# Value product with the features on partitions, probabilities scaled on GpSimd, in a float32 attention and mixture-of-experts kernel on one Trainium2 core

## What is computed

```python
scores = scale * np.matmul(q, k.transpose(0, 1, 3, 2))
scores = np.where(masks[None, :, :, :], scores, -1000000000.0)
scores = scores - np.max(scores, axis=-1, keepdims=True)
attn = np.exp(scores)
attn = attn / (np.sum(attn, axis=-1, keepdims=True) + 1e-09)
out = np.matmul(attn, v)
...
x = attn_out.transpose(0, 2, 1, 3).reshape(B * S, H * D)
x = _moe_ref(x=x, **moe_kwargs)       # x @ w_in, h * tanh(softplus(h)), @ w_out
return _moe2_ref(x=x, **moe2_kwargs)  # one of eight experts for each row
```

## Time and profile before

| | |
|---|---|
| three runs | 965.39, 967.73, 969.03 us, median 967.73 us |
| profiled execution, first to last instruction | 966.3 us |
| busy: PE, DVE, ACT, POOL | 860.1, 766.8, 390.3, 354.2 us |
| matmuls | 5778 |

### The profile page before, as it was taken

One profiled execution on the slowest core, in us unless ns is written; L12 is line 12 of the kernel. 1 busy time (PEld: TensorE's weight loads), 2 busy tenths in 40 slices (PEclk: granted clock), 3 DMA queues, 4 the chain that ended last, 5 costly groups with the idle time before them and its releaser, 6 DMA issues.

```text
span 966.3 us, 17706 instructions
## 1 busy us (share of the span) xinstructions
PE 860.1 (89%) x5778; PEld 788.7 (82%) x5779; DVE 766.8 (79%) x1658; ACT 390.3 (40%) x1043; POOL 354.2 (37%) x281
## 2 busy tenths in 40 slices
PE   5777899999998999998899889996599999999995
PEld 4676798888988988888898889995488888888884
DVE  5899988989888888887888988775657776778752
ACT  5565454545435445454544544445131122311300
POOL 4757432333243334333334333325414324423400
PEclk9789999999999999999999999997699999999998
DMA  9332411121121112112111211203473364645210
GB/s 326 132 128 85 140 32 46 59 64 45 41 68 42 54 50 67 42 42 67 42 47 61 62 42 64 90 1 120 164 267 126 125 214 133 188 160 191 71 44 22
DMA packets 34121, 91.00 MB, mean 94 GB/s; under 512 B 4224, under 2 KB 4672, under 8 KB 34048
## 3 DMA queue, kind: packets, MB, share of 16 engines
q1 hardware_dynamic: 18608, 48.31, 15.4%
q10 hardware_dynamic: 12224, 31.46, 9.7%
q0 software_dynamic: 3216, 10.26, 3.0%
HBM read 77.65 MB, written 12.37 MB: 93 GB/s over the span
## 4 chain that ended last, share of the span: by engine, by line
PE 39%; DVE 38%; ACT 12%; issue 9%; DMA 2%; DVEq 0%; SPq 0%; POOL 0%; ACTq 0%; POOLq 0%
PE ps_h L498 13%; PE acc L517 12%; DVE u_sb L806 6%; DVE u_sb L804 5%; DVE neg_max L754 5%; ACT probs L611 5%; DVE h_sb L812 4%; PE ps_h L389 4%; DVE row_max L747 3%; DVE probs L743 3%; PE acc L404 3%; DVE g_hi L817 2%; ACT u_sb L624 2%; ACT u_sb L626 2%; PE misc L416 2%
## 5 line engine op out<-in xcount | busy, mean ns | idle before, releaser
L1084 POOL TENSOR_TENSOR g_lo<-h_sb,g_hi 128x288 fp32r<-128x288 f32 x128 | 103.0, 805 | 296.8 <-DVE g_hi L817 296.8
L404 PE MATMUL acc<-g_hi,w_hi 128*128 128x288 f32 x512 | 161.4, 315 | 0.9 <-POOL g_lo L1084 0.9
L389 PE MATMUL ps_h<-xT_hi,w_hi 128*128 128x288 f32 x512 | 158.9, 310 | 0.0
L389 PE MATMUL ps_h<-xT_hi,w_lo 128*128 128x288 f32 x512 | 155.5, 304 | 0.0
L389 PE MATMUL ps_h<-xT_lo,w_hi 128*128 128x288 f32 x512 | 155.3, 303 | 0.0
L404 PE MATMUL acc<-g_lo,w_hi 128*128 128x288 f32 x512 | 152.7, 298 | 0.0
L404 PE MATMUL acc<-g_hi,w_lo 128*128 128x288 f32 x512 | 152.2, 297 | 0.0
L624 ACT ACTIVATE u_sb<-u_sb 128x288 f32<-128x288 f32 x128 | 56.8, 444 | 180.7 <-DVE u_sb L806 178.8
L1079 POOL TENSOR_TENSOR stage_lo<-stage,qk_hi 128x704 fp32r<-128x704 f32 x52 | 88.4, 1701 | 103.8 <-ACT qk_hi L603 103.7
L611 ACT ACTIVATE probs<-probs,neg_max 72x104 f32<-72x104 f32 (+1 forms) x224 | 84.6, 379 | 98.6 <-DVE neg_max L754 98.6
L806 DVE SCALAR_TENSOR_TENSOR u_sb<-u_sb 128x288 f32<-128x288 f32 x128 | 99.6, 778 | 4.4
(11 more groups left out here) (139 smaller groups left out, 2011.5 us busy)
## 6 DMA issues: line engine op xcount, KB each, us to landing
stage<-in_pack SPq DMA_DIRECT2D x57, 480.0 KB, 3.4
stage<-in_w ACTq DMA_DIRECT2D x32, 512.0 KB, 7.8
stage_w<-in_w ACTq DMA_DIRECT2D x28, 512.0 KB
x_row<-dispatched_x SPq DMA_DIRECT2D x22, 258.0 KB, 2.6
w_loaded<-in_w_in SPq DMA_DIRECT2D x8, 512.0 KB, 5.9
w_loaded<-in_w_out SPq DMA_DIRECT2D x8, 512.0 KB, 7.1
dispatched_x<-x2T SPq DMA_DIRECT2D x8, 258.0 KB, 4.7
stage_w<-in_w SPq DMA_DIRECT2D x4, 512.0 KB
```

The costliest lines, as they stand in the source:

```text
L389: mm = pe.matmul(ps_h[f % 2][:, 0:CHUNK], w[:, o + k * PIECE:o + k * PIECE + P], x[:, par, k, :], start=(k == 0 and w is w_hi and x is xT_hi),
L404: mm = pe.matmul(acc[d][:, 0:CHUNK], w[:, o + d * P:o + (d + 1) * P], g[:, f % RING, :], start=(f == 0 and w is w_hi and g is g_hi), stop= ...
L1084: nc.gpsimd.tensor_tensor(g_lo[:, f % RING, :], h_sb[:, f % RING, :], g_hi[:, f % RING, :].bitcast(F32), ALU.subtract).then_inc(g_lo_done, 1)
```

## The change

The value product is turned round: the values (64 features of a head) are the stationary operand and `probsT` moves, so the result has features on partitions and needs no transpose. Two heads share a pair of partition halves, with the layout that the transposed `o_sb` had. Since queries are then columns, 1/sum can't be applied to the product as one number for each partition; it is applied to `probs` ahead of the transpose, by POOL (`normalise`). The transposes L377 and `o_sb` are gone. 1/sum is now made in the even step (`invert_sums`), behind that step's rounding L817 and ahead of the clamp L804, and waits for the exponentials. The PE transposes of the probabilities wait for POOL's product (`weights_ready`) where they waited for the exponentials (`probs_ready`). `misc` has one use less for each group.

```diff
             def transpose_probs(a, par, g, use):
                 nq, nk = spec(g)
-                pe.wait_ge(probs_ready, a * NG + g + 1)
+                pe.wait_ge(weights_ready, a * NG + g + 1)
...
             def values(a, g, use, bank):
+
                 nq, nk = spec(g)
                 pe.wait_ge(misc_read, use)
                 for h in range(HG):
-                    mm = pe.matmul(bank[0:nq, h * DH:(h + 1) * DH], probsT[0:nk, h * QP:h * QP + nq],
+                    half, j = h % 2 * DH, h // 2
+                    mm = pe.matmul(bank[half:half + DH, j * P:j * P + nq],
                                    group_place(qkv, w_loaded, a, g)[0:nk, V_OFF + h * DH:V_OFF + (h + 1) * DH],
-                                   start=True, stop=True, skip_group_check=True)
-                mm.then_inc(misc_full, 1)
-
-            def transpose_out(g, use, bank):
-                nq, _ = spec(g)
-                pe.wait_ge(misc_read, use)
-                for j in range(2):
-                    mm = pe.transpose(bank[:, j * P:j * P + nq], o_sb[0:nq, j * P:(j + 1) * P], ident[0:nq, 0:nq])
+                                   probsT[0:nk, h * QP:h * QP + nq], start=True, stop=True, skip_group_check=True)
                 mm.then_inc(misc_full, 1)
...
-            def normalise(a, par, g, use, bank):
+            def invert_sums(a, par, g):
                 nq, _ = spec(g)
                 G = a * NG + g
                 r = (par + g) % 2
+                dve.wait_ge(probs_ready, G + 1)
                 nc.vector.tensor_scalar(sums_eps[0:nq, r, :], sums[0:nq, r, :], 1e-9, None, ALU.add).then_inc(eps_done, 1)
                 dve.wait_ge(eps_done, G + 1)
                 nc.vector.reciprocal(rsum[0:nq, r, :], sums_eps[0:nq, r, :]).then_inc(rsum_done, 1)
-                dve.wait_ge(rsum_done, G + 1)
-                dve.wait_ge(misc_full, use + 1)
-                nc.vector.tensor_tensor(o_sb[0:nq, :].rearrange("q (h d) -> q h d", h=HG),
...
                     if mlp and (st >= 1 or later):
                         make_g(n - 1, (st - 1) % NF)
+                    if attn and st % 2 == 0 and g < NG:
+                        invert_sums(c + 1, apar, g)
                     if mlp:
                         make_n(n, st)
                     if routing and st - 1 in ROUTE_STEPS[0:3]:
                         choose(c - 1, ROUTE_STEPS.index(st - 1))
-                    if attn and st % 2 == 1 and g < NG:
-                        normalise(c + 1, apar, g, u0 + uses[("V", g)], misc)
...
+            invert_sums(0, 0, 0)
             for g in range(NG):
+                if g + 1 < NG:
+                    invert_sums(0, 0, g + 1)
                 copy_probsT(g, PROLOGUE[("T", g)])
...
+            def normalise(a, par, g):
+
+                nq, nk = spec(g)
+                r = (par + g) % 2
+                pool.wait_ge(rsum_done, a * NG + g + 1)
+                nc.gpsimd.tensor_tensor(probs[0:nq, r, :, 0:nk], probs[0:nq, r, :, 0:nk],
+                                        rsum[0:nq, r, :].unsqueeze(2).to_broadcast([nq, HG, nk]), ALU.mult
+                                        ).then_inc(weights_ready, 1)
...
                     if st >= 1 or later:
                         subtract_g(c * NF + st - 1, (st - 1) % NF)
+                    if attn and st % 2 == 0 and st // 2 < NG:
+                        normalise(c + 1, 1 - par, st // 2)
 
             W_FIRST = NG - 2
             pool.wait_ge(qk_lo_done, 2)
             for g in range(NG):
+                normalise(0, 0, g)
                 if g + 2 < NG:
                     subtract_qk(0, 0, g + 2)
```

More of the change, by code:

```diff
@@ L66, in misc_uses @@
     for st in range(NF):
-        if attn and st % 2 == 0 and 1 <= st // 2 <= NG:
-            order.append(("X", st // 2 - 1))
         if route and st in ROUTE_STEPS:
@@ L73, in misc_uses @@
     return {u: i for i, u in enumerate(order)}
-PROLOGUE = {u: i for i, u in enumerate([("T", 0), ("V", 0)] + [(u, h) for g in range(1, NG) for u, h in
-                                                                (("T", g), ("X", g - 1), ("V", g))] + [("X", NG - 1)])}
+PROLOGUE = {(u, g): 2 * g + i for g in range(NG) for i, u in enumerate("TV")}
 def build(nc, pack, masks, eye, tri, small, gates, w_in, w_out, w1, w2, out):
@@ L123, in build @@
         probsT = sb("probsT", [P, HG * QP], F32, phase1)
-        o_sb = sb("o_sb", [QP, HG * DH], F32, phase1)
         pad_rows = x2T[:, 1:3, :].rearrange("p r n -> p (r n)")[:, 0:ROW]
@@ L184, in build @@
         rsum_done = sem("rsum_done")
+        weights_ready = sem("weights_ready")
         misc_full = sem("misc_full")
@@ L233, in uses_before @@
             if isinstance(c, int) and c == 0:
-                return len(ROUTE)
-            return 2 * len(ROUTE) - len(SUB) + len(SUB) * c
+                return len(PROLOGUE)
+            return len(PROLOGUE) + len(ROUTE) - len(SUB) + len(SUB) * c
         row_banks = [ps_h[0][0:TT, :], ps_h[1][0:TT, :], ps_s[0:TT, :, :].rearrange("p h k -> p (h k)")]
-        TAIL_BASE = 2 * len(ROUTE) + (NCHUNK - 2) * len(SUB) + len(TAIL)
+        TAIL_BASE = len(PROLOGUE) + len(ROUTE) + (NCHUNK - 2) * len(SUB) + len(TAIL)
         def group_place(ring, weights, a, g):
@@ L437, in round_ @@
                         gemm1(c, par, st)
-                    if attn and st % 2 == 0 and 1 <= g <= NG:
-                        transpose_out(g - 1, u0 + uses[("X", g - 1)], misc)
                     if attn and st % 2 == 1 and g < NG:
@@ L454, in _ @@
             for g in range(NG):
-                transpose_probs(0, 0, g, PROLOGUE[("T", g - 1)] + 1 if g else None)
+                transpose_probs(0, 0, g, PROLOGUE[("T", g)] - 1 if g else None)
                 if g + 2 < NG:
                     scores(0, 0, g + 2)
-                if g:
-                    transpose_out(g - 1, PROLOGUE[("V", g - 1)] + 1, ps_h[(g - 1) % 2])
                 values(0, g, PROLOGUE[("T", g)] + 1, acc[g % 2])
-            transpose_out(NG - 1, PROLOGUE[("V", NG - 1)] + 1, ps_h[(NG - 1) % 2])
             pe.wait_ge(consts_in, 16 * 3)
@@ L769, in normalise @@
                 nc.vector.reciprocal(rsum[0:nq, r, :], sums_eps[0:nq, r, :]).then_inc(rsum_done, 1)
-                dve.wait_ge(rsum_done, G + 1)
-                dve.wait_ge(misc_full, use + 1)
-                nc.vector.tensor_tensor(o_sb[0:nq, :].rearrange("q (h d) -> q h d", h=HG),
-                                        bank[0:nq, 0:HG * DH].rearrange("q (h d) -> q h d", h=HG),
-                                        rsum[0:nq, r, :].unsqueeze(2).to_broadcast([nq, HG, DH]), ALU.mult
-                                        ).then_inc(misc_read, 1)
             def split_x(a, par, g, use, bank):
@@ L897, in round_ @@
                     if attn and st % 2 == 0 and 1 <= g <= NG:
-                        split_x(c + 1, apar, g - 1, u0 + uses[("X", g - 1)], misc)
+                        split_x(c + 1, apar, g - 1, u0 + uses[("V", g - 1)], misc)
                     if mlp:
@@ L936, in _ @@
                     row_maxima(0, 0, g + 2)
-                if g:
-                    split_x(0, 0, g - 1, PROLOGUE[("X", g - 1)], ps_h[(g - 1) % 2])
-                normalise(0, 0, g, PROLOGUE[("V", g)], acc[g % 2])
-                if g + 2 < NG:
                     negate_maxima(0, 0, g + 2)
-            split_x(0, 0, NG - 1, PROLOGUE[("X", NG - 1)], ps_h[(NG - 1) % 2])
+                split_x(0, 0, g, PROLOGUE[("V", g)], acc[g % 2])
             dve.wait_ge(consts_in, 16 * 3)
```

## The result

Four runs of the changed kernel took 985.89, 988.24, 991.85 and 992.24 us, median 990.05; four of the kernel before, beside them, 966.56 in the median. The ratio is 1.024, interval 1.018 to 1.030: slower by 2.4%. The forecast was 974.5 with a range of 960 to 993. The profiled execution took 988.24 us, its span is 986.4.

What follows compares the result with a forecast made beforehand. PE and DVE share the chain, 39% and 38%; the price is set by which DVE instruction meets which POOL instruction. 6.1 + 13.5 - 12.8 = +6.8 on the 966.3 span gives 973.1, plus 1.4 makes 974.5 us; range 960 to 993.

Steps and rivals of the forecast that it cites:

- -12.8: Rounds 1 to 6: net change in us, from a per-round sum of -2.1 times 6.
- The leading rival: Whole kernel: DVE held as summed, 974.5 us, own range 968 to 982; chance 0.45.
- PE's transposes wait for the product: Steady pairs: transposes wait until L817 + 2.0 us, DVE needs them only at L817 + 2.9; priced at 0.
- second rival: Maxima lose their race with stage_lo: 1.15 us back for 2 or 3 groups in 6 rounds, 984 to 994; chance 0.25.
- Gain of the turned product: Steady pairs: maxima begin at once, ahead of stage_lo; gain 1.19 us a pair, 1.09 for 96 queries.
- Loss beside the product: Steady pairs: L804 held through g_lo and product; loss 1.02 us for 72 queries, 1.23 for 96.
- third rival: Faster: L804 let in between POOL instructions, maxima keep their lead, PE's shorter work counts; 963 us or less; chance 0.18.
- The product's size: POOL's new product: 1.08 us for 416 columns, 1.29 for 512, bounds 0.8 and 2.4.
- the dear product: POOL's product takes 2.0 us rather than 1.1 in 56 groups: +50 at most, +25 if half covered, 1000; chance 0.12.
- Round 0: Weight piece follows the product at once, L804 meets g_lo, product and piece in a row: +13.5 us.
- Start-up: First transposes wait for the product, POOL's low parts and weight pieces queue behind it: +6.1 us, bounds 4 and 8.
- PE 0: PE's shorter work, transposes gone and value product's moving side wider: taken as 0 us, bounds -4 and +4.

Runs made afterwards that it cites:

- nobody_waits: Changed kernel, but POOL's product reads the mask and writes an unread spare tile, and PE's transposes wait for the exponentials; attention unscaled; 987.75 us, rounds 1 to 6 437.6.
- no_scaling: Changed kernel without POOL's product of probs and 1/sum, transposes waiting for the exponentials; attention unscaled; 939.51 us, rounds 1 to 6 410.5.
- piece_behind_g: Changed kernel with POOL subtracting the weight piece behind g_lo instead of ahead of it in odd steps of round 0; 980.64 us, ratio 1.017 to the kernel before.
- scaling_on_dve: Changed kernel with the product of probs and 1/sum made by DVE behind the reciprocal instead of by POOL; 954.49 us, ratio 0.990 to the kernel before.

## Why the prediction came out as it did

Direction and range held; the number was 15.6 us low, and the range held by 3 us, in part by luck. It summed +6.1, +13.5 and -12.8 (its own -2.1 times 6 is -12.6); the stages gave +12.1, +10.8, +0.1 and, in the rest, -2.9, together the 20.1 us between the two spans. The rest is nearly the same code, and lies within what the kernels here differ by in it. So start-up and rounds came out 6.0 and 12.9 above the sum, round 0 and rest 2.7 and 2.9 below. The leading rival's own range, 968 to 982, missed. Point by point:

- **The failed step: PE's transposes wait for the product, "so I price this at 0".** nobody_waits puts 20.5 us on it in rounds 1 to 6. The forecast had seen the chain as its second rival (maxima that lose their race with `stage_lo`, in 2 or 3 groups a round), and that is what happened in kind: two groups a round lose it. Group 4 loses it by 0.04 us, in no_scaling and nobody_waits too, as it feared of routing's small work. The other, a 96-query group, loses it through the wait, at 2.9 us (1.4 at full clock) where 1.15 were given. The 9.0 us of group 0, and the clock that makes a PE wait of 2 us cost another 1.4 in the matmuls behind it in five of six pairs, it had not seen.
- **Gain of the turned product, rounds 1 to 6.** The prediction's parts (1.09 twice, 1.19 three times, 2.1 and 1.0, in six rounds) sum to 53; no_scaling measured 47.4. Right in sum. Most of the gap is group 4, whose pairs gave 0.4 us in all for 7.1, since its L741 stays held; group 3 gave 14.9 for 12.6: no wait of L408 for x, and its pair takes 10.1 us in the changed kernel from one mask addition to the next where it took 11.3 to 13.6.
- **Loss beside the product, rounds 1 to 6.** Priced at 1.23 twice, 1.02 three times and 1.2, six times: 40. Measured 27.0, with another instruction held. It was to be L804, held through `g_lo` and product; the clamp was let in at that boundary and the polynomial stood beside the product. A clamp of under 0.9 us was the forecast's sign of its third rival, the faster one; the sign came true and the gain did not, since polynomial and wait took it.
- **The product's size**: 1.10 and 0.94 us for a forecast of 1.29 and 1.08. It falls by less than the columns do; the dear product (2.0) is out.
- **Round 0**: 10.8 us for 13.5, the mechanism nearly right (product and weight piece in a row, piece_behind_g gives 7.3 of it back; the other 3.5 were not looked into), the held line again the polynomial.
- **Start-up**: 12.1 for 6.1. The hand count had L741 blocked by one POOL instruction at a time; it stood through two, the low part of q and k and the weight piece, 3.3 to 3.5 us, three times over. nobody_waits (56.8) shows that PE's wait has no part in it, and scaling_on_dve (50.8) that 6.5 us go with the product's place on POOL. The means of the clock (0.72 for 0.86) explain little: the scores' matmuls of 256 columns took 0.41 us in both start-ups, but for one group of before at 0.28.
- **Clock and PE**: PE 0 was its own term with bounds of 4. On PE's side the eight matmuls of the value product went from 0.67 to 0.47 us for 72 queries, 30% less and not the half, which bought nothing off the path.
